# The first network's tiles as one stream: the last two sets of output sums move into the next tile

## The reference

```python
# q, k, v: 4 batches x 8 heads x 768 tokens x 48; beta: 4 x 8 x 768
k_n = k / (norm(k) + 1e-6)
for t in range(768):                        # delta rule, one state per batch and head
    y[t]   = q[t] @ state                   # read before the update
    v_old  = state^T k_n[t]
    state += beta[t] * outer(k_n[t], v[t] - v_old)
x  = heads of y side by side                # 3072 x 384
h  = x @ w_in                               # 384 x 2048
g  = where(h >= 1, h, where(h <= -1, 0, (h + 1)**2 / 4))
x2 = g @ w_out                              # 2048 x 384
xn = x2 / sqrt(mean(x2**2) + 1e-6) * rms_g
y  = (silu(xn @ w_gate) * (xn @ w_val)) @ w_out2     # 384 x 1536, 1536 x 384
```

## Time and profile before

| | |
|---|---|
| runs | 1110.57, 1110.81, 1114.39 us, median 1110.81 |
| profiled execution | 1107.6 us, of which 1105.8 are its span |
| TensorE, matmuls | 1050.9 us busy (95%), 10956 instructions |
| VectorE | 577.5 us busy (52%), 977 instructions |
| ScalarE | 431.6 us busy (39%), 693 instructions |
| first network's tiles 0 to 4 | 89 to 565 us |
| last tile | 565 to 641 us |
| second network | 641 us to the end |

### The profile page before, as it was taken

The page is one execution under the profiler, slowest core; times in us unless marked ns, Lnnn a source line. Parts: engine busy times, 40 slices in busy tenths (PEclk is TensorE's granted clock), DMA queues, the critical chain, the costliest instruction groups (busy, mean ns, idle before and its releaser), DMA issues.

```text
span 1105.8 us, 24421 instructions
## 1 busy us (share of the span) xinstructions
PE 1050.9 (95%) x10956; PEld 851.8 (77%) x10956; DVE 577.5 (52%) x977; ACT 431.6 (39%) x693; POOL 9.6 (1%) x20
## 2 busy tenths in 40 slices
PE   4889899999999899999979999999999999999996
PEld 3467677777777677767767888888888888888885
DVE  4848858858848947862335634333324324233222
ACT  3644444453464364454446644222232132232121
POOL 1000000000000000000000000000000000000000
PEclk9879999999999999999989999999999999999999
DMA  7704001400410230020030212010100200100101
GB/s 204 199 5 111 7 4 35 111 3 2 121 25 3 77 69 3 2 87 2 3 143 29 86 58 86 29 29 1 44 14 1 58 1 1 29 1 1 29 1 28
DMA packets 18904, 48.06 MB, mean 43 GB/s; under 512 B 2416, under 2 KB 9200, under 8 KB 17648
## 3 DMA queue, kind: packets, MB, share of 16 engines
q1 hardware_dynamic: 18800, 46.51, 15.5%
HBM read 37.06 MB, written 9.44 MB: 42 GB/s over the span
## 4 chain that ended last, share of the span: by engine, by line
PE 85%; DVE 10%; ACT 2%; issue 2%; DMA 1%; DVEq 0%; SPq 0%; ACTq 0%
PE bank L635 20%; PE hps L1123 16%; PE acc L1136 16%; PE acc L654 10%; PE hps L635 7%; PE hps L654 3%; DVE outer L910 2%; DVE inv L914 2%; PE bank L1041 1%; PE bank L1052 1%; PE bank L1064 1%; PE bank L1030 1%; PE bank L1011 1%; PE bank L1087 1%; PE bank L1076 1%
## 5 line engine op out<-in xcount | busy, mean ns | idle before, releaser
L555 ACT ACTIVATE g<-bank 128x512 f32<-128x512 f32 x72 | 43.1, 599 | 254.7 <-PE bank L635 141.7
L1136 PE MATMUL acc<-g1h,w2h 128*128 128x512 f32 x288 | 121.6, 422 | 14.5 <-DVE g1l L975 14.5
L1123 PE MATMUL hps<-xh,w1h 128*128 128x512 f32 x288 | 121.1, 420 | 6.6 <-DVE g L968 5.0
L1136 PE MATMUL acc<-g1h,w2l 128*128 128x512 f32 x288 | 114.8, 399 | 0.0
L1136 PE MATMUL acc<-g1l,w2h 128*128 128x512 f32 x288 | 114.6, 398 | 0.0
L1123 PE MATMUL hps<-xh,w1l 128*128 128x512 f32 x288 | 114.4, 397 | 0.0
L1123 PE MATMUL hps<-xl,w1h 128*128 128x512 f32 x288 | 114.2, 397 | 0.0
L830 ACT ACTIVATE g1h<-g 128x512 fp32r<-128x512 f32 x96 | 60.6, 632 | 130.7 <-DVE g L968 118.0
L975 DVE TENSOR_TENSOR g1l<-g,g1h 128x512 fp32r<-128x512 f32 x96 | 66.1, 689 | 74.0 <-ACT g1h L830 73.7
L968 DVE SCALAR_TENSOR_TENSOR g<-hps,g 128x512 f32<-128x512 f32 x96 | 65.9, 686 | 68.6 <-ACT g L824 68.3
L821 ACT ACTIVATE g<-hps,half_c 128x512 f32<-128x512 f32 x96 | 65.8, 685 | 77.5 <-PE hps L1123 77.2
(11 more groups left out here) (159 smaller groups left out, 2031.8 us busy)
## 6 DMA issues: line engine op xcount, KB each, us to landing
kqT<-kq SPq DMA_DIRECT2D x24, 384.0 KB, 6.4
v_in<-v SPq DMA_DIRECT2D x6, 768.0 KB, 4.2
k_in<-k SPq DMA_DIRECT2D x6, 768.0 KB, 4.4
x2d<-x2s SPq DMA_DIRECT2D x18, 256.0 KB, 2.3
x2t<-x2d SPq DMA_DIRECT2D x6, 768.0 KB, 6.2
y<-y_t SPq DMA_DIRECT2D x48, 96.0 KB, 2.2
stage<-w_in SPq DMA_DIRECT2D x4, 768.0 KB, 11.3
stage<-w_out SPq DMA_DIRECT2D x4, 768.0 KB, 4.5
```

What stands on the lines that cost most here:

```text
L1123: last = pe.matmul(hps[f % 2][:, :], wt[:, kk, P * f:P * f + P], xx[:, kk, :], start=(kk == 0 and e == 0), stop=(kk == KD - 1 and e == 2))
L1136: last = pe.matmul(acc[j][:, :], wt[:, f, P * j:P * j + P], gg[:, f % 2, :], start=(f == 0 and e == 0), stop=(f == NF1 - 1 and e == 2))
```

## The change

1. `ffn(n)` no longer drains at its end. Its first steps contain the rest of the tile before (`back`): `gh` and `gl` of f = 15, the output sets of f = 14 and 15, and the `x2` copies at f = 1. `ffn_end` gives this rest once, for the last tile, and `second_network` puts it around its first unit: `gv` 0 stands ahead of the last two output sets.
2. The transposes XT stand ahead of the three thirds of the last input set. Their evictions are a unit of their own, `XE`, behind which `h` of f = 15 stands on ScalarE, and which waits for the last input set on TensorE.
3. GQ of a chunk k moves from the end of body k - 1 to the start of body k, for every chunk; `LAST` goes from 0.90 to 0.94. In the first body, which has 90 network units instead of 96, both GQ come ahead of the first input set.
4. SP loads `x2t` for two tiles when the queries of chunk 4 have been used, and issues the first two loads of weights ahead of the stores of tile 4; the stores of each tile come later in the loop. `x2t`, `rms` and `rinv` lie at another place for that.
5. Two waits of ScalarE on `s_gl` and `s_o` are added in the first two units of the second network.

```diff
@@ ffn
+    def back(f, by):
+        return divmod(NF1 * n + f - by, NF1)
     out = []
...
+    for f in range(NF1):
+        out += [("h0", n, f), ("gh", *back(f, 1)), ("h1", n, f), ("gl", *back(f, 1)), ("h", n, f)]
+        out += [(kind, *back(f, 2)) for kind in ("o0", "o1", "o")]
+        if f == 1:
+            out += [("x2", n - 1, j) for j in range(KD)]
+        out += [("g", n, f)]
+    return [u for u in out if u[1] >= 0]
+def ffn_end():
+    n = NSTEP - 1
+    out = [("gh", n, NF1 - 1), ("gl", n, NF1 - 1)]
+    for f in (NF1 - 2, NF1 - 1):
+        out += [(kind, n, f) for kind in ("o0", "o1", "o")]
     return out + [("x2", n, j) for j in range(KD)]
@@ serial
-    if 0 < c < NSTEP - 1:
-        out += [("GQ", c + 1, hf) for hf in range(HALVES)]
@@ first_body
-    return out + [("XT", 0, n) for n in range(KD)], ahead
+    return out + [(kind, 0, n) for kind in ("XT", "XE") for n in range(KD)], ahead
-LAST = 0.90
+LAST = 0.94
@@ next_body
-    if k == 1:
-        ev += [(0.02 + 0.04 * hf, ("GQ", 1, hf)) for hf in range(HALVES)]
+    ev += [(0.02 + 0.04 * hf, ("GQ", k, hf)) for hf in range(HALVES)]
...
-    tail = {("h", k - 1, NF1 - 1): 0, ("o0", k - 1, NF1 - 3): 1, ("o", k - 1, NF1 - 3): 2}
-    out, done = [], 0
+    tail = {("h0", k - 1, NF1 - 1): 0, ("h1", k - 1, NF1 - 1): 1, ("h", k - 1, NF1 - 1): 2}
+    out, done = [], 0 if k > 1 else NFF - len([e for e in ffn(0) if e[0] in FFN_PE])
...
-        out.append(e)
         if e in tail:
             out.append(("XT", k, tail[e]))
+        if e == ("h", k - 1, NF1 - 1):
+            out += [("XE", k, n) for n in range(KD)]
+        out.append(e)
@@ second_network
+                if f == 0:
+                    end = ffn_end()
+                    out = out[:1] + end[:2 + KD] + out[1:] + end[2 + KD:]
@@ build
+        x2t = [sb(f"x2t{i}", [P, KD, T]) for i in range(2)]
+        rms = sb("rms", [P, T])
+        rinv = sb("rinv", [P, T])
         wgh = sb("wgh", [P, KD, F2], F32R)
...
@@ second_scalar, silu
+                    if n == 0 and f < 2:
+                        act.wait_ge(s_gl, NF1 * NSTEP - 1 + f)
...
+                    else:
+                        act.wait_ge(s_o, NF1 * NSTEP - 1 + f)
@@ sync
                         load_v(c)
-                        if c > 1:
-                            x2_store(c - 2)
...
                         load_k(c)
+                        if c > 1:
+                            x2_store(c - 2)
...
-                    x2_store(NSTEP - 2)
+                    sp.wait_ge(p_y, HALVES * (NSTEP - 1))
+                    for n in range(2):
+                        load_x2(sp, n)
                     sp.wait_ge(s_xl, NSTEP * KD)
                     load_w2(sp, 0)
-                    for n in range(2):
-                        load_x2(sp, n)
-                    for r in range(1, len(W2_ORDER)):
+                    load_w2(sp, 1)
+                    x2_store(NSTEP - 2)
+                    for r in range(2, len(W2_ORDER)):
                         load_w2(sp, r)
@@ scalar
-                        elif kind == "XT":
+                        elif kind == "XE":
                             act.wait_ge(p_xt, KD * c + hf + 1)
+                            if c:
+                                act.wait_ge(s_h, NF1 * c)
```

More of the change, by code:

```diff
@@ L85, in serial @@
 def serial(c):
-    out = [(kind, c, hf) for hf in range(HALVES) for kind in ("KS", "U", "QS", "PU", "KU")]
-    if 0 < c < NSTEP - 1:
-        out += [("GQ", c + 1, hf) for hf in range(HALVES)]
-    return out
+    return [(kind, c, hf) for hf in range(HALVES) for kind in ("KS", "U", "QS", "PU", "KU")]
 NPIECE = NCHUNK * PIECES
@@ L331, in build @@
         stage2 = sb("stage2", [P, 2, F2])
-        x2t = [sb(f"x2t{i}", [P, KD, T]) for i in range(2)]
         x2sq = sb("x2sq", [P, KD, T])
-        rms = sb("rms", [P, T])
-        rinv = sb("rinv", [P, T])
         pr = sb("pr", [P, 2, T])
@@ L809, in attention @@
                                                bank_of(("QS", c, hf), j)[:, 0:BIG], ACT.Copy).then_inc(s_y, 1)
-                        elif kind == "XT":
+                        elif kind == "XE":
                             act.wait_ge(p_xt, KD * c + hf + 1)
-                            act.activation(xh[:, hf, :], bank_of(u)[:, :], ACT.Copy).then_inc(s_xh, 1)
+                            if c:
+                                act.wait_ge(s_h, NF1 * c)
+                            act.activation(xh[:, hf, :], bank_of(("XT", c, hf))[:, :], ACT.Copy).then_inc(s_xh, 1)
                     def forward(u):
@@ L863, in _ @@
                         second_scalar(act, u)
+                        forward(u)
                 @block.vector
@@ L957, in attention @@
                                 dve.tensor_tensor(st, st, bank_of(u, m)[:, 0:BIG], ALU.add).then_inc(s_state, 1)
-                        elif kind == "XT":
+                        elif kind == "XE":
                             dve.wait_ge(s_xh, KD * c + q + 1)
-                            dve.tensor_tensor(xl[:, q, :], bank_of(u)[:, :], xh[:, q, :].bitcast(F32), ALU.subtract)\
+                            dve.tensor_tensor(xl[:, q, :], bank_of(("XT", c, q))[:, :], xh[:, q, :].bitcast(F32), ALU.subtract)\
                                 .then_inc(s_xl, 1)
```

## The result

The changed kernel takes 1095.6 us (median of four runs, 1094.25 to 1096.52) beside 1111.77 for the kernel before, measured with it (median of four, 1110.57 to 1114.39): a ratio of 0.985, 95% interval 0.9828 to 0.9873. The forecast was 1095.5. It rested on 1110.8 for the kernel before, so that the hit to 0.1 us is partly luck: 15.3 us were forecast, and the medians differ by 16.2. The profiled execution took 1096.28 us, its span is 1094.5 with a mean granted clock of 0.984. The whole agrees; the terms under it agree less well, and in part their errors cancel.

What follows compares the result with a forecast made beforehand. The prediction took TensorE's pauses and slow clock as the bound, with VectorE the most-contended engine between two trace rows. Its terms, -9.5 + 2.2 - 7.2 - 0.8 = -15.3, took the 1110.8 us median to 1095.5, range 1091 to 1100.

Steps and rivals of the forecast that it cites:

- Part 1: Ends of tiles 0 to 4: moving output sums of f = 14 and 15 into the next tile nets -9.5 us.
- Part 2: Tile ends: input transposes ahead of the last input set, their evictions behind it, cost 0.
- Part 3: First tile: both GQ units of chunk 1 ahead of the first input sets cost +2.2 us.
- Rival B: TensorE's clock falls at the new waits, four falls of 1.6 us: 1101.9 us, chance 0.07.
- Part 4: Last tile: loading `x2t` early removes ScalarE's wait and TensorE's pause and slow matmuls, -7.2 us.
- Part 5: End of first network: gate and value sets ahead of the last two output sets, -0.8 us.
- A: VectorE holds tiles 0 to 3 altogether, so they win nothing: 1103.1 us, chance 0.16.
- C: All pauses vanish and the first tile catches up, 23 us won: 1087.8 us, chance 0.12.
- D: VectorE's debt makes tiles 0 to 3 each wait 5.5 us more than the walk: slower, 1117.5 us, chance 0.03.

Runs made afterwards that it cites:

- The variant without the stream: Changed kernel with each tile's last two output sets back at the tile's own end and `LAST` back at 0.90: 1101.32 us, ratio 0.9909 to the kernel before.
- the second profile: Changed kernel measured and profiled again on another chip, no edit: 1094.31 us, ratio 0.9852 to the kernel before.
- the later GQ: Changed kernel with the second GQ unit of chunks 2 to 5 at 0.11 of the tile instead of 0.06: 1094.34 us, ratio 0.9852 to the kernel before.
- two more edits: Changed kernel with chunk 1's units moved back as before and left-over inversion steps of chunks 2 to 5 starting 0.04 of a tile later: 1089.07 us.
- the variant with the x2 rows alone: Kernel before with only the early loads of the first two x2 tiles and their buffer layout: 1104.66 us, ratio 0.9938.

## Why the prediction was right, and where it was not

- **Part 1, the tile ends (forecast -9.5).** Right in mechanism and nearly in size. The pauses of the earlier trace rows are gone, and the new waits lie where the walk through the two queues put them: behind tile 0 1.17 for the mask and 0.57 for `g`, with 0.26 each 2.3 us against 2.45; behind tile 2 1.3 against 1.35; behind tile 1 0.6 against 1.2; behind tile 3 none is listed, and 0.3 is lost ahead of the second GQ, against 0.45. Measured -11.4 (0.5 + 3.5 + 2.9 + 2.7, and 9.0 less the 7.2 of the x2 rows). Of the 1.9 that the term was too small, 0.7 is a third pause after tile 3 in the kernel before, which the prediction left out (0.44 with its 0.26):
```profile
483.58 0.49 PE L1136 MATMUL acc<-g1h,w2h 128*128 128x512 f32 x1 [0.44 <-DVE g1l L975]
```
The variant without the stream brings the pauses back, 12.5 us with the new waits gone.
- **Part 2 (0).** TensorE has no wait for the copies (L979 or its ScalarE counterpart) at any tile end. Shown only as an absence.
- **Part 3, the first tile (forecast +2.2).** The sign was right and the two first waits too: I had the first input set 7.9 us after the first transpose, it came at 8.74. The mis-sized term is the clock. The walk priced all at 2.4 GHz. In the trace the second GQ lost 0.8, and the eleven matmuls of input sets from 98.52 to 103.27 took 4.75 us instead of 2.6, 2.1 lost. The 1.4 us wait of set 2 for `g` did not come, since the slow matmuls took its place: 2.2 + 0.8 + 2.1 - 1.4 = 3.7, measured 3.6 and, in the second profile, 2.5; putting the placing back won 2.8 to 3.9. Rival B was thus right in one place, the start of the first tile; in the second profile the clock is down already behind the first wait (2.07 us), and only three matmuls of input sets still take 0.63.
- **Part 4, x2 rows (-7.2).** Right, alone 7.2 in its stretch and 6.2 (4.2 to 9.6) in the runs.
- **Part 5 (-0.8).** Wrong. I took the 0.7 us in the earlier trace rows for the first y sum without looking up its place in time; it is the last. No time went there on either side.
- **The sum.** -15.3 forecast, -15.0 in the profiles from the first transpose on, -16.2 between the medians. Part 1's gain was forecast 1.9 too small, Part 3's price 1.4 too small, and Part 5's gain of 0.8 was none. That they cancel is luck. The step from the profiled execution to the median (+3.2) fits the early transpose of that execution (86.11, near the low end of what was seen): adding the difference back to the median took that chance out again. That this is the reason was not tested.
- **Rivals.** A: refuted as a total, by the table (the stretches of tiles 0 to 3 won 9.6 us, where it gave none) and by moving VectorE's steps, which won 2.4 to 2.9 more; it holds as a local debt behind tile 0, where the later GQ won nothing. C: the kernel that comes near to it, 1089.07, needed two more edits. D: no wait of that kind was seen.

Left open: what decides the clock in the first 86 us, and how often it falls behind the waits of the later GQ; its one profile shows such a fall, while its median is that of the changed kernel.

## What to carry to other kernels

A placing by counts moves everything when the count's start moves: after such a change, look at what the other engines' queues hold at the first place where the new and the old count differ. An engine that is busy three quarters of the time can still hold another; ask which of its instructions nobody needs yet and put these behind those that are waited for. Here that won as much as making them lighter. And a wait in a list has a place in time: look it up before it becomes a term of a sum.

## What the runs showed of the hardware

A pause of TensorE of about 2 us lowered its clock in some of these profiles and not in others. 1.77 us at the end of tile 3 left it at 2.4 GHz in the kernel before and took it to 1.2 GHz in the variant with the x2 rows alone, as 1.77 us behind tile 0 did in the variant with the later GQ; of the four pauses of 2.0 to 2.2 us in the variant without the stream three have a granted clock of 0.98 in their stretch and one 1.00. A wait of 1.42 us ahead of the first input set did not do it in the rows above; 2.77 us ahead of the second GQ did. Behind 2.06 us the next GQ ran at full speed in one profile of the changed kernel (1.16 us), and in the other it ran at 1.96 behind 2.07. Such a fall cost 1.4 us in the variant with the x2 rows alone and 2.9 in the first tile of the changed kernel, about as much as the pause itself or more.
